# Local attention before two feed-forward layers: V's key spans at one distance in two transfers a unit, and the low parts of two w_in pieces given to other places

## The reference

```python
mask = np.abs(pos[:, None] - pos[None, :]) < 4          # a query sees 7 keys
scores = np.where(mask, scale * (q @ k.T), -1e9)
out = np.repeat(softmax(scale * (q_d @ k_d.T)) @ v_d, 4, axis=2) + softmax(scores) @ v
x = out.transpose(0, 2, 1, 3).reshape(2304, 512)
h = x @ w_in;  x = (h * tanh(softplus(h))) @ w_out       # w_in 512 x 2048, w_out 2048 x 512
h = x @ w2_in; y = layernorm(h * softmax(h)) * g @ w2_out
```

## Time and profile before

| | us |
|---|---|
| median of 3 runs | 710.22 (708.73 to 711.64) |
| the profiled execution | 708.51 |
| its span, first to last instruction | 706.7 |
| TensorE busy | 679.5 (96%) |
| DVE, ACT, GpSimd busy | 366.6, 261.2, 183.7 |
| chain that ended last | PE 84%, POOL 6%, DVE 4%, issue 3%, ACT 1%, DMA 1% |

### The profile page before, as it was taken

One profiled execution on the slowest core, in us unless ns is written; L12 is line 12 of the kernel. 1 busy time (PEld: TensorE's weight loads), 2 busy tenths in 40 slices (PEclk: granted clock), 3 DMA queues, 4 the chain that ended last, 5 costly groups with the idle time before them and its releaser, 6 DMA issues.

```text
span 706.7 us, 12612 instructions
## 1 busy us (share of the span) xinstructions
PE 679.5 (96%) x5098; PEld 629.5 (89%) x5098; DVE 366.6 (52%) x675; ACT 261.2 (37%) x583; POOL 183.7 (26%) x221
## 2 busy tenths in 40 slices
PE   6887889999999999999999999999989999999998
PEld 5776679999999999999999999999768888888886
DVE  7998867542223222323232332564796667756671
ACT  5787774322111211121121122135564544435441
POOL 5998820000000000000000000574535434354100
PEclk9999999999999999999999999999999999999999
DMA  7887683000000000000000030002100000000001
GB/s 240 228 251 228 191 305 150 1 0 1 1 1 1 1 0 1 1 1 1 0 1 1 1 119 1 1 1 86 35 16 16 30 31 16 16 31 30 31 16 45
DMA packets 25657, 37.51 MB, mean 53 GB/s; under 512 B 2944, under 2 KB 13184, under 8 KB 25472
## 3 DMA queue, kind: packets, MB, share of 16 engines
q1 hardware_dynamic: 25600, 36.72, 16.4%
HBM read 31.99 MB, written 4.72 MB: 52 GB/s over the span
## 4 chain that ended last, share of the span: by engine, by line
PE 84%; POOL 6%; DVE 4%; issue 3%; ACT 1%; DMA 1%; SPq 0%; POOLq 0%; DVEq 0%; ACTq 0%
PE psum L690 28%; PE psum L676 28%; PE psum L786 12%; PE psum L763 11%; PE psum L772 2%; POOL half_v L502 2%; POOL half_qk L491 1%; POOL prob L510 1%; POOL ylo L553 1%; PE psum L662 1%; DMA qkT<-kT_dram 1%; POOL vd L503 1%; POOL qd L493 1%; PE psum L646 1%; DVE so L1315 1%
## 5 line engine op out<-in xcount | busy, mean ns | idle before, releaser
L1212 DVE CAST ghi<-g_sb 128x384 fp32r<-128x384 f32 x96 | 39.6, 413 | 245.3 <-PE psum L690 188.4
L903 ACT ACTIVATE g_sb<-psum 128x384 f32<-128x384 f32 x96 | 47.1, 491 | 292.3 <-PE psum L676 288.1
L676 PE MATMUL psum<-xhi,whi 128*128 128x384 f32 x384 | 129.6, 338 | 1.7 <-ACT g_sb L903 0.7
L676 PE MATMUL psum<-xhi,wlo 128*128 128x384 f32 x384 | 129.0, 336 | 0.0
L690 PE MATMUL psum<-ghi,wlo 128*128 128x384 f32 x384 | 129.0, 336 | 0.0
L676 PE MATMUL psum<-xlo,whi 128*128 128x384 f32 x384 | 129.0, 336 | 0.0
L690 PE MATMUL psum<-ghi,whi 128*128 128x384 f32 x384 | 129.0, 336 | 0.0
L690 PE MATMUL psum<-glo,whi 128*128 128x384 f32 x384 | 129.0, 336 | 0.0
L525 POOL TENSOR_TENSOR t<-raw 128x1024 f32<-128x1024 f32 x1 | 2.6, 2615 | 350.1 <-PE psum L690 350.1
L676 PEld LDWEIGHTS psum<-xhi,whi 128*128 128x128 f32 x384 | 72.2, 188 | 2.8 <-ACT g_sb L903 1.2
L690 PEld LDWEIGHTS psum<-glo,whi 128*128 128x128 f32 x384 | 72.2, 188 | 0.1
(11 more groups left out here) (124 smaller groups left out, 1062.0 us busy)
## 6 DMA issues: line engine op xcount, KB each, us to landing
wraw<-w_dram SPq DMA_DIRECT2D x12, 512.0 KB, 7.9
qkT<-qT_dram SPq DMA_DIRECT2D x16, 288.0 KB, 3.8
qkT<-kT_dram SPq DMA_DIRECT2D x16, 288.0 KB, 4.9
out_dram<-ob SPq DMA_DIRECT2D x18, 256.0 KB, 2.0
v<-v_dram SPq DMA_DIRECT2D x16, 256.0 KB, 3.0
vw<-v_dram SPq DMA_DIRECT2D x32, 128.0 KB, 3.0
wraw<-w_dram SPq DMA_DIRECT2D x16, 256.0 KB, 6.2
raw<-w_dram SPq DMA_DIRECT2D x1, 2048.0 KB, 7.2
```

The costliest lines, as they stand in the source:

```text
L676: ins = nc.tensor.matmul(bank, a[:, w], b[:, kdx, :], start=(kdx == 0 and n == 0), stop=(kdx == KD - 1 and n == 2))
L903: nc.scalar.activation(g_sb[:, f % HR, :], psum[:, HB1 + f % HB, 0:N1], ACT.Mish).then_inc(g_ok, 1)
L1212: nc.vector.tensor_copy(ghi[:, f % GR, :], g_sb[:, f % HR, :]).then_inc(ghi_ok, 1)
```

## The change

`window` no longer clips, so that all spans begin 3 keys ahead of their block and lie 58 keys apart; a unit's spans of one `jp` are loaded in one transfer of five. A span that reaches outside the unit reads its neighbour's keys, whose probabilities are zero; only unit 0's first and unit 15's last span are cut and loaded by themselves, and what they lack in unit 0 is set to zero. q and k get 12 columns of zeros (`SEQP`, 588 a row) for the same reason, and the first span's three keys ahead of k's row are the zeros behind q's. All blocks share one form of the band; columns outside are masked by two small memsets.

GpSimd makes the low part of w_in's piece 1 at its step 15, behind the pooling of unit 14's V, with a semaphore of its own. DVE makes that of piece 0 at step 15, behind the last `subtract_local` and ahead of the last `split_x`.

```diff
 def window(i, jp):
-    return min(max(first_query(i, jp) - (POOLF - 1), 0), SEQ - KW)
+    return first_query(i, jp) - SHIFT
...
-        qkT = sb("qkT", [P, RQ, 2, SEQ])
+        qkT = sb("qkT", [P, RQ, 2, SEQP])
...
-        VW_DMAS = 4
+        def window_loads(u):
+            return 2 * (u // 2 + 1) + (1 if u % 2 == 0 or u == UNITS - 1 else 0)
...
             def load_windows(u):
                 par = u % 2
                 wait(sp, l_valued, u - 1)
+                if u == 0:
+                    sp.wait_ge(rest_ok, 5)
                 v_u = v_d[u]
-                for jp, i0, n in ((0, 0, 1), (0, 1, NP - 1), (1, 0, NP - 1), (1, NP - 1, 1)):
+                for jp in range(2):
+                    i0, i1 = 0, NP
+                    if u == 0 and jp == 0:
+                        sp.dma_start(vw[SHIFT:KW, par, 0, :], v_u[0:KW - SHIFT]).then_inc(ld_vw[par], 16)
+                        i0 = 1
+                    if u == UNITS - 1 and jp == 1:
+                        i1 = NP - 1
+                        k0 = window(i1, 1)
+                        sp.dma_start(vw[KW:KW + SEQ - k0, par, i1, :], v_u[k0:SEQ]).then_inc(ld_vw[par], 16)
                     src = bass.AP(v_u.tensor, v_u.offset + window(i0, jp) * P,
-                                  [[P, KW], [PSTEP * P, n], [1, P]])
-                    sp.dma_start(vw[jp * KW:(jp + 1) * KW, par, i0:i0 + n, :], src).then_inc(ld_vw[par], 16)
+                                  [[P, KW], [PSTEP * P, i1 - i0], [1, P]])
+                    sp.dma_start(vw[jp * KW:(jp + 1) * KW, par, i0:i1, :], src).then_inc(ld_vw[par], 16)
...
                 if u > 0:
                     pool_values(u - 1)
+                if u == UNITS - 1:
+                    pool.wait_ge(wi_hi, 2)
+                    nc.gpsimd.tensor_tensor(in_piece(wlo, 1), in_piece(wraw, 1), in_piece(whi, 1).bitcast(F32),
+                                            ALU.subtract).then_inc(wi_lo_pool, 1)
...
-                if t == 0:
-                    pe.wait_ge(wi_lo, f + 1)
+                if t == 0 and f == 1:
+                    pe.wait_ge(wi_lo_pool, 1)
+                elif t == 0:
+                    pe.wait_ge(wi_lo, f if f > 1 else 1)
...
-            pe.wait_ge(rest_ok, 3)
+            pe.wait_ge(rest_ok, 5)
...
+            nc.vector.memset(qkT[:, :, :, SEQ:SEQP], 0.0).then_inc(rest_ok, 1)
+            nc.vector.memset(vw[0:KW, 0, 0, :], 0.0).then_inc(rest_ok, 1)
...
-                nc.vector.tensor_copy(maskb[rows, 0:NB:NB - 1, :],
-                                      band[rows, h, 0, :].unsqueeze(1).broadcast_to([HD, 2, KW])).then_inc(mask_ok, 1)
-                nc.vector.tensor_copy(maskb[rows, 1:NB - 1, :],
-                                      band[rows, h, 1, :].unsqueeze(1).broadcast_to([HD, NB - 2, KW]))\
+                nc.vector.tensor_copy(maskb[rows], band[rows, h, :].unsqueeze(1).broadcast_to([HD, NB, KW]))\
                   .then_inc(mask_ok, 1)
+            dve.wait_ge(mask_ok, 2)
+            nc.vector.memset(maskb[:, 0, 0:SHIFT], MASKED).then_inc(mask_ok, 1)
+            nc.vector.memset(maskb[:, NB - 1, SEQ - window(NP - 1, 1):KW], MASKED).then_inc(mask_ok, 1)
...
                 if u == UNITS - 1:
+                    weights_in_low(0)
                     split_x(0, KD - 1)
...
-                if UNITS - 2 <= u < UNITS:
-                    weights_in_low(u - UNITS + 2)
```

More of the change, by code:

```diff
@@ L28 @@
 KW = 64
-QB = KW - 2 * (POOLF - 1)
+SHIFT = POOLF - 1
+QB = KW - 2 * SHIFT
 NP = 5
@@ L43 @@
 QPAD = (NPB - 1) * PB + HD
+SEQP = SEQ + 12
 TOK = BATCH * SEQ
@@ L95, in window @@
 def window(i, jp):
-    return min(max(first_query(i, jp) - (POOLF - 1), 0), SEQ - KW)
-def first_row(i, jp):
-    return min(first_query(i, jp), SEQ - KW)
+    return first_query(i, jp) - SHIFT
 def wait(eng, sem, value):
@@ L153, in program @@
         half_v = sb("half_v", [P, 2, 2 * P])
-        band = sb("band", [P, 2, 2, KW], BF16)
+        band = sb("band", [P, 2, KW], BF16)
         assert top[0] <= whi_end, (top[0], whi_end)
@@ L277, in program @@
         wi_lo = sem("wi_lo")
+        wi_lo_pool = sem("wi_lo_pool")
         xlo_ok = sem("xlo_ok")
@@ L408, in _ @@
                     wait(sp, p_scored, s + 1 - RQ)
-                    sp.dma_start(qkT[:, s % RQ, 0, :], qT_d[s]).then_inc(ld_qk[s % RQ], 16)
-                    sp.dma_start(qkT[:, s % RQ, 1, :], kT_d[s]).then_inc(ld_qk[s % RQ], 16)
+                    sp.dma_start(qkT[:, s % RQ, 0, 0:SEQ], qT_d[s]).then_inc(ld_qk[s % RQ], 16)
+                    sp.dma_start(qkT[:, s % RQ, 1, 0:SEQ], kT_d[s]).then_inc(ld_qk[s % RQ], 16)
                 if s > 2:
@@ L468, in _ @@
                                     base=0, pattern=[[-1, P]], channel_multiplier=1).then_inc(ident_ok, 1)
-            shift = POOLF - 1
             own(nc.gpsimd.memset(band[:], 0.0))
             own(nc.gpsimd.affine_select(out=band[:], in_=band[:], compare_op=ALU.is_ge, fill=MASKED,
-                                        base=shift, pattern=[[-KW, 2], [shift, 2], [-1, KW]],
-                                        channel_multiplier=1))
+                                        base=2 * SHIFT, pattern=[[-KW, 2], [-1, KW]], channel_multiplier=1))
             nc.gpsimd.affine_select(out=band[:], in_=band[:], compare_op=ALU.is_ge, fill=MASKED,
-                                    base=shift, pattern=[[KW, 2], [-shift, 2], [1, KW]],
-                                    channel_multiplier=-1).then_inc(band_ok, 1)
+                                    base=0, pattern=[[KW, 2], [1, KW]], channel_multiplier=-1).then_inc(band_ok, 1)
             own(nc.gpsimd.memset(mhalf[:], -0.5))
@@ L489, in pool_queries_keys @@
                 halves = half_qk[:].rearrange("p a (i r) -> p a i r", r=2)
-                four = qkT[:, u % RQ].rearrange("p a (i r) -> p a i r", r=4)
+                four = qkT[:, u % RQ, :, 0:SEQ].rearrange("p a (i r) -> p a i r", r=4)
                 own(nc.gpsimd.tensor_tensor(halves[:, 0:n], four[:, 0:n, :, 0:2], four[:, 0:n, :, 2:4], ALU.add))
@@ L597, in score_local @@
             def score_local(u):
-                par = u % 2
+                qk = qkT[:, u % RQ].rearrange("p a s -> p (a s)")
                 pe.wait_ge(ld_qk[u % RQ], 32 * (u // RQ + 1))
@@ L607, in score_local @@
                     for jp in range(2):
-                        q0, k0 = first_row(i, jp), window(i, jp)
+                        q0, k0 = first_query(i, jp), window(i, jp)
                         for h in range(2):
@@ L611, in score_local @@
                             ins = nc.tensor.matmul(psum[out, SLB + jp, i * KW:(i + 1) * KW],
-                                                   qkT[rows, u % RQ, 0, q0:q0 + KW], qkT[rows, u % RQ, 1, k0:k0 + KW],
+                                                   qk[rows, q0:q0 + KW], qk[rows, SEQP + k0:SEQP + k0 + KW],
                                                    start=False, stop=(i == NP - 1))
@@ L652, in value_local @@
                 pe.wait_ge(l_copied, u + 1)
-                pe.wait_ge(ld_vw[par], 16 * VW_DMAS * (u // 2 + 1))
+                pe.wait_ge(ld_vw[par], 16 * window_loads(u))
                 wait(pe, x_ok, u)
@@ L660, in value_local @@
                             rows = slice(h * HD, (h + 1) * HD)
-                            q0 = i * P + (h ^ jp) * HD + first_query(i, jp) - first_row(i, jp)
+                            q0 = i * P + (h ^ jp) * HD
                             ins = nc.tensor.matmul(psum[rows, OB + jp, i * QB:i * QB + n], vw[keys, par, i, rows],
@@ L1086, in pool_with_one @@
                 par = u % 2
-                nc.vector.tensor_reduce(dst[:, par, 0:POOLED], qkT[:, u % RQ, a, :].rearrange("p (i r) -> p i r", r=POOLF),
+                nc.vector.tensor_reduce(dst[:, par, 0:POOLED], qkT[:, u % RQ, a, 0:SEQ].rearrange("p (i r) -> p i r", r=POOLF),
                                         AX.X, ALU.add).then_inc(ok, 1)
```

## The result

The changed kernel takes **703.23 us** (median of 5 runs, 703.12 to 704.94), the kernel before on the same chip 710.22 (707.72 to 711.64): a ratio of 0.9912, 95% interval 0.9886 to 0.9937, or 7.0 us less. The profiled execution took 703.15 us, 5.36 less than the profiled one of before; in other comparisons the kernel before had medians of 708.62 (35 runs), 709.31 (27), 708.82 (18) and 707.72 (13). Against those 703.23 is 4.5 to 6.1 less. So some 4.5 to 6 us are the kernel's gain; the rest of the 7.0 is the draw of that first comparison. A part of the draw goes with TensorE's granted clock, told at the end: of these 93 runs of before, 44 have a mean of 0.999 or 1.00 and a median of 707.7, and the other 49, with a lower one, a median of 709.6.

What follows compares the result with a forecast made beforehand. SyncE's late window issues were taken to bound units 9 to 13, GpSimd's pace the rest of the attention. 2.56 + 2.46 - 1.2 = 3.8 us off the median 710.22 gave 706.4 us, 8-in-10 range 704.6 to 709.8.

Steps and rivals of the forecast that it cites:

- The bound: In the attention V's windows land late because SyncE issues them late: 5.77 us a unit against GpSimd's 5.16.
- the third period: GpSimd's normalisation from unit 9 to unit 13, 23.21 us before; forecast to take 20.65, 2.56 less.
- the 5.5 us of the earlier trace: TensorE's idling ahead of the local product with V, in 57 to 84 us, laid to late windows; forecast gone.
- To the last subtraction: From unit 13's normalisation to the end of unit 15's subtraction: 7.14 us in place of 9.60, 2.46 less.
- the first rival: "The landings don't come earlier": 23.21 stays, 1.74 us saved before the subtraction, 1.2 lost behind it; 709.7; chance 0.17.
- Behind the subtraction: From unit 15's subtraction to the second hidden block, 4.48 us before: 1.2 us more taken, bounds 0.24 to 2.1.
- rest: What follows the moved split up to the second hidden block: 4.42 - 0.38 = 4.04 us.
- the 3.00 of idling: GpSimd's normalisation waiting for the denominators; taken to cover GpSimd's new piece, which uncovered would cost 1.3 us.
- The median: Last step of the sum: the same 3.8 us taken off the median of the runs, 710.22, gives 706.4.
- The landings don't come earlier: If the DMA engines, not SyncE, set when V's windows land: 0.5 us less, 709.7 (same); chance 0.17.
- Rows at the new distance are slower: q's and k's SBUF rows, 2352 bytes apart, take the DMA engines longer: 4.6 us more, 714.8; chance 0.06.
- The tail doesn't do what it says: GpSimd's piece isn't covered (1.3) on top of 2.1 behind the subtraction: 1.6 us less, 708.6; chance 0.09.

Runs made afterwards that it cites:

- V's sum on TensorE: Changed kernel, in every second unit the second half of V's pooling taken from GpSimd and made by TensorE: 707.75 us, ratio 0.9996.
- before again: The kernel before once more, unchanged: 709.06 us, ratio 1.0004.
- the splits alone: The kernel before with only the two moved splits added, four window transfers kept: 707.85 us, ratio 0.9988.
- the windows alone: The changed kernel without its two moved splits, V's windows still in two transfers: 705.07 us, ratio 0.9955.
- piece 0 alone: The changed kernel with piece 1's low part back on DVE, piece 0's staying behind the last subtraction: 703.62 us.
- one small transfer more: The changed kernel with one more 2 KB transfer of V a unit into a spare tile: three runs 703.12 to 703.49 us, seven 705.31 to 707.06.
- the changed kernel again: The changed kernel once more, unchanged: 703.9 us, ratio 0.9932.

## Why the prediction was wrong, point by point

**The bound: right.** SyncE was late, and two transfers fewer a unit were enough to end it. They brought the third period to 20.65 us (forecast: 2.56 less; measured 2.56). With the transfers back in number, whether four useful ones or two of 2 KB, the lag is back with SyncE's waits near zero. The issue cost is flat, as taken: 0.62 us for five windows. One reading was too simple: of the 5.5 us of the earlier trace rows, 1.12 stood in the middle of a local product, at 77.07, where no late window can be the reason.

**To the last subtraction: right.** 2.46 forecast, 2.44 measured. How I split it was wrong: I had the 1.74 of the moved split come even if SyncE's lag stayed. On top of the windows the splits do bring 1.66 of it, but alone only some 0.7 of the whole time, so the 1.74 of the first rival was not to be had.

**Behind the subtraction: the step that failed in the sum.** I took 1.2 us more and it was 0.14 less, an error of 1.34. The step reads "I take 1.2 more, nearer the upper part, since the piece, the moved split and x's split are all ready within one microsecond there." They were, and they did collide, but not on the path. The pooling took 1.07 in place of 0.73 us, x's split 1.09, GpSimd's piece 1.61, where the kernel with V's sum on TensorE has 1.30 for it. The moved split began at 84.64, 0.21 us ahead of the pooling, and went through in 0.68: the first block began 0.70 behind the subtraction, not some 1.6. That is 0.94 of the error: the bare duration of 0.68, the lower bound that I had passed over, was the right price. The other 0.40 is the "rest" that I took as 4.04 us of fixed work: TensorE now gets through it in 3.64 (85.42 to 89.06). In the kernel before it holds further idling, 0.24 us for x's eviction ahead of unit 13's local product among it, and the block that started later had its inputs ready. GpSimd's piece was ready at 87.48, the last denominators at 87.55: it hid behind 0.07 us, not behind the 3.00 of idling that I named, because the denominators came earlier too.

The rule of the Trainium skill that stood beside this step (SBUF — State Buffer, section Who interferes with whom: the loser waits for the whole instruction of the other) agrees with the durations above. The same section says that the order of issue decides which of the two waits, and I had left that half out; it decided the sum. In each pair here the one that began later was the longer one, the pooling behind the moved split first of all, which agrees.

**The median: the second step that failed.** From the profiled 704.7 I went to 706.4 by taking 3.8 off the median, that is, I let the changed kernel keep the 1.7 us by which before's median lay above its profile. It has no such offset, 703.23 against 703.15. I had not asked where the 1.7 came from. The runs show two sources, and both are smaller in the changed kernel. One is the clock: 49 of the 93 runs of before stand below a mean of 0.999, some 1.9 us above the others, and three of eleven of the changed kernel. The other is left at 0.999 or 1.00, where the runs of before still go from 706.55 to 710.39 and seven of eight of the changed kernel from 703.12 to 703.28; that this is SyncE's lag, gone with the change, fits the periods but no run shows it by itself. Of the 3.2 us between forecast and time, 1.55 are the sum (1.34 and 0.24 at the start, less 0.04 on the periods and the stretch to the subtraction) and 1.62 this step. About one of these 1.62 is the draw of the first comparison, 710.22 against 707.72 to 709.31 in the others.

**The rivals.** "The landings don't come earlier" did not happen: with the same bytes the third period came back to 20.65. The Trainium skill's sentence that initiating is usually small beside the DMA itself (DMA: Bandwidth & Descriptors, section Issuing engines are not separate DMA queues) holds for one transfer here, 0.62 against 3.9 us, and is no guide for a queue that issues eight a unit end to end: two issues of 2 KB a unit cost 4.1 us. "Rows at the new distance are slower" is excluded: with four transfers at the new distance the kernel is at 707.28, not above before. "The tail doesn't do what it says" did not happen; it does 1.7 us.

## What to carry to other kernels

A DMA queue can be bound by the issuing engine's time for each transfer, whatever it moves (SyncE without waits in a long stretch is the sign), and this is read apart from the DMA engines' share. Merging transfers helps only against the first, and only down to the pace of the next bound. When several instructions collide behind an event, price the one that the end waits for: who begins first pays little. And a stretch of "fixed work" taken from a trace should be searched for idling before it is carried over; a spread of runs should be carried over only if its cause is known and stays. And before a profile is compared with another, the granted clock of the stretch belongs beside both.

## What the runs showed of the hardware beyond that

**Stops at instruction packets.** SyncE's issues of 1.0 to 2.2 us in the kernel before, for which no view gave a reason, fall together with packets of 16 KB on queue q8, kind "instruction": the issue at 67.08 of the earlier trace rows with one at 67.00 to 68.87 us, that of k at 74.33 to 76.23 with one at 74.31 to 75.86. From 8 to 92 us all thirteen issues longer than 0.9 us overlap such a packet, and all but one of the fourteen packets overlap such an issue. The DMA view of 66.9 to 68.9 us in that kernel:

```profile
q8 instruction: 1, 0.02, 5.9%
```

TensorE's stops of 0.7 to 2.4 us in the middle of a group ended 1.2 to 1.8 us after such a packet had passed, in the profiles of before, of before again, of the splits alone and of seven of the other kernels; that of the windows alone has one of 0.77 behind a group's first weight load. In the changed kernel's first profile and in those of piece 0 alone and of V's sum on TensorE there is none, though packets pass there too. The profile of the kernel with one small transfer more has one of these, and another of 2.13 us ahead of a turn whose input ACT had made by 84.06, whose place ACT had emptied by 84.54, and whose packet had passed at 85.47 (with four transfers and with two small ones more the same turn comes 1.58 and 1.59 us late):

```profile
79.88 0.44 PE L684 MATMUL psum<-probT,vw 64*64 64x58 f32 x11 [0.73 <-issue]
...
87.06 0.77 PE L648 MATMUL psum<-ident,pprob 112*128 112x112 f32 x6 [2.13 <-issue]
```

That such stops make the upper groups of runs of the changed kernels, some 1.5 to 2 us above the lower, is read from three profiles, each of a run in the upper group, and no run was made that changes the packets. When a packet stops an engine and when not stays open.

**TensorE's clock.** The other thing in the upper groups is the granted clock. In the changed kernel's eleven runs three of the four slowest have a mean of 0.998, all others 1.00; with one small transfer more the three of 706.99 to 707.06 have 0.997 or 0.998 and the four of 705.31 to 705.88 have 1.00. In the profiles the stretch at the lower level stands at another place each time: in 12 to 18 us for the changed kernel again, in 60 to 64 us for before again. What makes the clock fall is not shown: in the changed kernel's first profile TensorE was busy for 1.82 of the 3.00 us from 12 to 15 us and kept 1.00, in the second, where it fell, for 1.83.
